# Attention and gated feed-forward on one core: probabilities times values in plain fp32, two heads side by side in PSUM, V loaded one pair ahead, the gate by the sigmoid

## The reference

```python
q_rot, k_rot = rotate(q), rotate(k)                  # rotary embedding
scores = q_rot @ k_rot.T / sqrt(64)
attn = softmax(scores)                               # over the keys
x = attn @ v                                         # 4 x 576 x 512 once the heads are joined
xn = (x - mean) / sqrt(var + 1e-6) * g_ln
x = x + relu(xn @ w_ch1) @ w_ch2                     # 512 -> 2048 -> 512
gate_pre = causal convolution of x over 5 tokens, one weight per tap and feature
out = (1 / (1 + exp(-gate_pre)) * (x @ w_val)) @ w_out
```

## Time and profile before

| | us |
|---|---|
| median of 3 runs | 957.6 (953.64 to 962.07) |
| the profiled execution | 955.4 |
| its span, first to last instruction | 953.5 |

### The profile page before, as it was taken

One profiled execution on the slowest core, in us unless ns is written; L12 is line 12 of the kernel. 1 busy time (PEld: TensorE's weight loads), 2 busy tenths in 40 slices (PEclk: granted clock), 3 DMA queues, 4 the chain that ended last, 5 costly groups with the idle time before them and its releaser, 6 DMA issues.

```text
span 953.5 us, 15415 instructions
## 1 busy us (share of the span) xinstructions
PE 826.4 (87%) x5104; PEld 785.0 (82%) x5104; DVE 579.0 (61%) x967; ACT 385.0 (40%) x927; POOL 251.6 (26%) x193
## 2 busy tenths in 40 slices
PE   0198888989888896399999999999999999999937
PEld 0187777878777785399999999999999999999936
DVE  6587978889798896353276138515732761375074
ACT  1386867778687784222210231122122102311121
POOL 4366768786687820100000000000000000000000
PEclk9999989999899999599999999999999999999977
DMA  8948686766868630541110020011001000100000
GB/s 244 251 119 187 156 180 160 195 164 160 192 148 186 156 87 25 166 148 43 37 32 1 25 76 1 1 56 45 1 13 59 29 1 26 53 1 1 34 0 33
DMA packets 69961, 83.18 MB, mean 87 GB/s; under 512 B 13088, under 2 KB 52256, under 8 KB 69920
## 3 DMA queue, kind: packets, MB, share of 16 engines
q1 hardware_dynamic: 69920, 82.61, 33.7%
HBM read 44.84 MB, written 9.44 MB: 57 GB/s over the span
## 4 chain that ended last, share of the span: by engine, by line
PE 50%; DMA 4%; DVE 3%; issue 1%; POOL 0%; ACT 0%; SPq 0%; DVEq 0%; ACTq 0%
PE ps_y L859 6%; PE ps_y L858 6%; PE ps_y L860 6%; PE ps_h L858 6%; PE ps_h L859 6%; PE ps_h L860 6%; DMA x_tok<-x_scratch 4%; PE ps_ring L858 4%; PE ps_ring L859 3%; PE ps_ring L860 3%; PE ps_ring L870 1%; DVE spare L1014 1%; PE ps_y L880 1%; DVE stats L976 0%; POOL rstd L828 0%
## 5 line engine op out<-in xcount | busy, mean ns | idle before, releaser
L993 DVE SCALAR_TENSOR_TENSOR h_lo<-ps_h,h_hi 128x384 fp32r<-128x384 f32 x96 | 53.2, 554 | 237.8 <-ACT h_hi L936 237.8
L936 ACT ACTIVATE h_hi<-ps_h 128x384 fp32r<-128x384 f32 x96 | 47.2, 492 | 322.8 <-PE ps_h L860 322.8
L410 PE MATMUL ps_scores<-qk 128*128 128x288 f32 (+1 forms) x320 | 104.0, 340 | 71.4 <-DMA qk<-parts 36.9
L585 DVE TENSOR_REDUCE neg_max<-ps_scores 128x1 f32<-128x576 f32 (+1 forms) x160 | 118.7, 750 | 29.3 <-PE ps_scores L411 26.2
L858 PE MATMUL ps_h<-normed_hi,w_hi 128*128 128x384 f32 x384 | 129.8, 338 | 1.4 <-DVE normed_lo L988 1.4
L858 PE MATMUL ps_y<-h_hi,w_hi 128*128 128x384 f32 x384 | 129.8, 338 | 0.0
L860 PE MATMUL ps_h<-normed_hi,w_lo 128*128 128x384 f32 x384 | 129.1, 336 | 0.0
L859 PE MATMUL ps_h<-normed_lo,w_hi 128*128 128x384 f32 x384 | 129.1, 336 | 0.0
L410 PEld LDWEIGHTS ps_scores<-qk 128*128 128x128 f32 (+1 forms) x320 | 59.3, 185 | 84.2 <-ACT probs L505 46.3
L860 PE MATMUL ps_y<-h_hi,w_lo 128*128 128x384 f32 x384 | 128.4, 334 | 0.0
L859 PE MATMUL ps_y<-h_lo,w_hi 128*128 128x384 f32 x384 | 128.3, 334 | 0.0
(11 more groups left out here) (98 smaller groups left out, 1695.6 us busy)
## 6 DMA issues: line engine op xcount, KB each, us to landing
raw<-in_qk SPq DMA_DIRECT2D x16, 576.0 KB, 4.1
swapped<-in_qk SPq DMA_DIRECT2D x64, 144.0 KB, 4.6
qk<-parts SPq DMA_DIRECT2D x32, 256.0 KB, 4.3
x_tok<-x_scratch SPq DMA_DIRECT2D x32, 256.0 KB, 3.2
qk<-parts SPq DMA_DIRECT2D x16, 432.0 KB, 4.0
qk<-parts SPq DMA_DIRECT2D x48, 144.0 KB, 4.2
qk<-parts SPq DMA_DIRECT2D x16, 288.0 KB, 5.2
out_dram<-spare SPq DMA_DIRECT2D x24, 192.0 KB, 1.9
```

The source lines that it names most:

```text
L410: pe.matmul(ps_scores[h][0:rows, c, 0:NC], lhs, qk[par][h][:, 1, cols], start=True, stop=False)
L585: dve.tensor_reduce(neg_max[0:rows, par, t, h:h + 1], ps_scores[h][0:rows, :, 0:NC], AX.XY, ALU.max, negate=True).then_inc(max_ready, 1)
L993: dve.scalar_tensor_tensor(out=h_lo[:, f % 2, :], in0=ps_h[f % 2][:, 0:CH], scalar=0.0, in1=h_hi[:, f % 2, :].bitcast(F32), op0=ALU.max, o ...
```

## The change

- `values` takes both heads at once, for one half of the queries. A product has 64 weight columns (V as it was loaded, fp32) and 288 queries (`pt`, fp32), and writes partitions 0 to 63 of `ps_out` for head 0 and 64 to 127 for head 1. The heads alternate. There are 20 such products a pair in place of 40.
- `part_hi` and `part_lo` become plain copies: HEAD0 by ScalarE (`keep_head0`), HEAD1 and TAILS by VectorE (`keep_head1`). `move_half` and `sum_halves` become one copy on ScalarE (`copy_out`), twice a pair. `values_hi` and `values_lo` are gone, and with them the waits of `prepare` on `v_ready`.
- `load_v` loads the next pair's V rather than that of two pairs ahead; the buffers are two, as before.
- The three orders are written anew: the values of a pair have two steps of 4 products and two of 6.
- The gate is one activation on ScalarE with the function Sigmoid.

```diff
 PE_ORDER = [
-    ("last turn", HEAD1, 3), ("last values", 0, 0), ("last rest", 0, 0),
-    ("scores", 0, 0), ("last turn", TAILS, 3), ("last turn", HEAD0, 4), ("last values", 1, 0),
+    ("last turn", HEAD1, 3), ("last values", 0, 0),
+    ("scores", 0, 0), ("last turn", TAILS, 3), ("last turn", HEAD0, 4), ("last rest", 0, 0),
     ("scores", 1, 0), ("last turn", HEAD1, 4), ("last turn", TAILS, 4),
-    ("scores", 0, 1), ("last rest", 1, 0), ("turn", HEAD0, 0),
+    ("scores", 0, 1), ("turn", HEAD0, 0),
     ("scores", 1, 1), ("turn", HEAD1, 0), ("turn", TAILS, 0),
-    ("scores", 0, 2), ("last values", 0, 1), ("last rest", 0, 1), ("turn", HEAD0, 1),
-    ("scores", 1, 2), ("turn", HEAD1, 1), ("last values", 1, 1),
-    ("scores", 0, 3), ("last rest", 1, 1), ("turn", TAILS, 1),
+    ("scores", 0, 2), ("last values", 1, 0), ("turn", HEAD0, 1),
+    ("scores", 1, 2), ("turn", HEAD1, 1), ("turn", TAILS, 1),
+    ("scores", 0, 3), ("last rest", 1, 0),
     ("scores", 1, 3), ("turn", HEAD0, 2), ("last tokens", 0, 0),
...
 def load_v(pair, par):
-                at_least(sp, v_ready, V_PARTS * (pair - 1))
+                at_least(sp, out_ready, 2 * (pair - 1))
...
-                if not isinstance(pair, int) or pair + 2 < PAIRS:
-                    load_v(pair + 2, par)
+                if not isinstance(pair, int) or pair + 1 < PAIRS:
+                    load_v(pair + 1, 1 - par)
...
             def prepare(j, par):
...
-                at_least(pool, v_ready, V_PARTS * (pair - 1))
...
             prepare(0, 1)
-            values_lo(0, 0)
             with pool.Fori(1, PAIRS // 2) as j:
                 prepare(j, 0)
-                values_lo(2 * j - 1, 1)
                 prepare(j, 1)
-                values_lo(2 * j, 0)
-            values_lo(PAIRS - 1, 1)
...
                 for n in range(2, FULL + 1) if rest else range(2):
-                    lhs = v_both[par][:, 2 * n + h, :] if n < FULL else v_tail[par][h][:, :]
-                    block_ = FULL * h + n if n < FULL else 2 * FULL
-                    pe.matmul(ps_out[:, 0:NC], lhs, pt_hi[:, block_, cols], start=(n == 0), stop=False)
-                    last = pe.matmul(ps_out[:, 0:NC], lhs, pt_lo[:, block_, cols], start=False, stop=(n == FULL))
+                    for h in range(2):
+                        lhs = v_main[par][:, 2 * n + h, :] if n < FULL else v_tail[par][h][:, :]
+                        block_ = FULL * h + n if n < FULL else 2 * FULL
+                        last = pe.matmul(ps_out[h * D:(h + 1) * D, 0:NC], lhs, pt[:, block_, cols],
+                                         start=(n == 0), stop=(n == FULL))
...
+            def copy_out(pair, c):
+                act.wait_ge(out_ready, 2 * pair + c + 1)
+                at_least(act, tokens_turned, 2 * pair)
+                act.copy(o_t[:, c * NC:(c + 1) * NC], ps_out[:, 0:NC]).then_inc(out_copied, 1)
...
-            def exps(c, k):
+            def sigmoid(c, k):
                 act.wait_ge(conv_step, KT * CONV * c + CONV * (k + 1))
-                act.activation(gate[:, k, :], gate[:, k, :], ACT.Exp, scale=-1.0).then_inc(exp_ready, 1)
+                act.activation(gate[:, k, :], gate[:, k, :], ACT.Sigmoid).then_inc(gate_step, 1)
...
-            def sigmoid(c, k):
-                done = 2 * KT * c + 2 * k
-                dve.wait_ge(exp_ready, KT * c + k + 1)
-                dve.tensor_scalar(gate[:, k, :], gate[:, k, :], 1.0, None, ALU.add).then_inc(gate_step, 1)
-                dve.wait_ge(gate_step, done + 1)
-                dve.reciprocal(gate[:, k, :], gate[:, k, :]).then_inc(gate_step, 1)
```

More of the change, by code:

```diff
@@ L53 @@
 ACT_ORDER = [
[L54 to L63, removed]
+    ("exps", 0, 0), ("last turn", HEAD0, 4),
+    ("exps", 1, 0), ("last out", 0, 0),
+    ("exps", 0, 1), ("turn", HEAD0, 0),
+    ("exps", 1, 1),
+    ("exps", 0, 2), ("turn", HEAD0, 1),
+    ("exps", 1, 2), ("last out", 1, 0),
+    ("exps", 0, 3),
+    ("exps", 1, 3), ("turn", HEAD0, 2),
+    ("exps", 0, 4),
+    ("exps", 1, 4), ("turn", HEAD0, 3),
 ]
@@ L66 @@
     ("scores", 0, 0), ("last turn", HEAD1, 3), ("last turn", TAILS, 3),
[L67 to L76, removed]
+    ("scores", 1, 0), ("last turn", HEAD1, 4),
+    ("scores", 0, 1), ("last turn", TAILS, 4),
+    ("scores", 1, 1), ("turn", HEAD1, 0),
+    ("scores", 0, 2), ("turn", TAILS, 0),
+    ("scores", 1, 2), ("turn", HEAD1, 1),
+    ("scores", 0, 3), ("turn", TAILS, 1),
+    ("scores", 1, 3), ("last tokens", 0, 0), ("turn", HEAD1, 2),
+    ("scores", 0, 4), ("turn", TAILS, 2), ("last tokens", 1, 0),
+    ("scores", 1, 4),
 ]
@@ L200, in attention @@
         inv = sb("inv", [P, NQ, 2])
-        half = sb("half", [P, NC])
         o_t = sb("o_t", [P, S])
@@ L238, in attention @@
         PREP = 6
-        V_PARTS = 3
+        V_LOADS = 3 * 16
         LOADS = 5 * 16
@@ L465, in walk @@
                         turn(pair, par, x, y)
-                    elif kind == "values":
-                        values(pair, par, x, y)
                     elif kind == "last turn":
@@ L470, in walk @@
                     elif kind == "last values":
-                        values(before, pb, x, y)
-                    elif kind == "rest":
-                        values(pair, par, x, y, rest=True)
+                        values(before, jb, pb, x)
                     elif kind == "last rest":
-                        values(before, pb, x, y, rest=True)
+                        values(before, jb, pb, x, rest=True)
                     elif kind == "last tokens":
@@ L488, in _ @@
             act.wait_ge(cleared_sums, 1)
-            def values_hi(pair, j, par):
-                act.wait_ge(v_loaded[par], 48 * (j + 1))
-                at_least(act, out_ready, 4 * (pair - 1))
-                apart(act, passed)
-                act.copy(v_both[par][:, :, 0:D], v_raw[par][:, :, :]).then_inc(v_hi_ready, 1)
-                for h in range(2):
-                    rows = slice(h * D, (h + 1) * D)
-                    act.copy(v_tail[par][h][rows, 0:D], v_raw_tail[par][rows, :]).then_inc(v_hi_ready, 1)
             def exps(pair, par, h, t):
@@ L503, in exps @@
                 act.wait_ge(max_ready, UNITS * pair + 2 * t + h + 1)
+                if h == 0:
+                    at_least(act, turned, GROUPS * pair + 3 * (t - 1))
+                    apart(act, passed)
                 p = probs[(par * NQ + t) % 2]
@@ L966, in _ @@
             run(act, {"slab": slab_part, "evict": evict, "up": relu, "keep": keep, "split": part_x,
-                      "sigmoid": exps, "gated parts": part_gated, "project": copy_out})
+                      "sigmoid": sigmoid, "gated parts": part_gated, "project": copy_out})
         @block.vector
@@ L1040, in _ @@
             run(dve, {"slab": slab_part, "stats": take_stats, "scale": scale, "evict": evict, "up": relu,
-                      "split": part_x, "conv": conv, "sigmoid": sigmoid, "gated": gated, "gated parts": part_gated})
+                      "split": part_x, "conv": conv, "gated": gated, "gated parts": part_gated})
 def program(nc, qk, v, cos, sin, ident, g_ln, w_ch1, w_ch2, w_val, conv_w, w_out, out):
```

118 lines of the change are left out of this document (43 added, 75 removed).

## The result

| | before | after |
|---|---|---|
| median of the runs, us | 958.08 (953.64 to 962.07, 4 runs) | 911.44 (907.43 to 914.28, 4 runs) |
| ratio, 95% interval | | 0.951 (0.945 to 0.957) |
| profiled execution, us | 955.4 | 914.28 |
| its span, us | 953.5 | 912.5 |
| first scores of pair 1 / pair 15 | 60.25 / 348.44 | 60.01 / 325.99 |

What follows compares the result with a forecast made beforehand. Attention was taken as bound by a two-pair loop through V, 20.0 us a pair. 955.4 - 32.5 (pairs 1 to 15) - 4.7 (rest of attention) - 10 (gate) = 908, so 910 for the median; range 893 to 986.

Steps and rivals of the forecast that it cites:

- The loop through V: Attention before: V split, V on POOL, prepare, stack and landing form a two-pair loop, 40.1 us, 20.0 a pair.
- The walk of 18.1: Time of one attention pair after the change, summed as 13.4 - 1.2 + 5.1 + 0.8 us.
- of the 1.2 us in which PE idles I take all away: Attention walk: lighter VectorE and ScalarE work removes all 1.2 us of TensorE idle time in a pair.
- The products: 5.1 plus 0.8: The 20 new values products take 5.1 us a pair, eight changes between 128 and 64 columns 0.8 more.
- The four streams: Values step: one plain fp32 product of 288 columns costs four streams through the array, 0.49 to 0.53 us.
- The overlap: Values step: both heads' products run in the array at once, 4.9 to 5.3 us a pair instead of 9.8 to 10.6.
- No overlap: Rival, chance 0.32: the two heads' values products follow each other; walk 22.6 us, total 982.
- In part: Rival, chance 0.14: only one head's last pass meets the other's first; walk 20.5 us, total 948.
- The supply binds: Rival, chance 0.10: supply of q and k, at least 17.0 us a pair, binds instead of V; walk 19.5, total 930.
- V one pair ahead, and the copies: Attention: loading V one pair ahead costs nothing; VectorE's copies cost the same as the subtractions they replace.
- Clock and feed-forward: Half-clock spells in attention cost 6 us before, 3 left; the feed-forward before its last keep was forecast unchanged.
- The gate: -10: End of the feed-forward: one Sigmoid on ScalarE beside the next convolution starts the last gated 10 us earlier.

Runs made afterwards that it cites:

- before_no_add: Kernel before with VectorE's addition of 1e-9 to the softmax sums left out: 962.85 us, 1.005 of before.
- v_split_early: Kernel before with ScalarE's split of V moved up, to behind the copies of tile 0: 954.15 us, 0.997 of before.
- no_add: Changed kernel with VectorE's addition of 1e-9 to the softmax sums left out: 898.53 us, 0.940 of before.
- one_column: no_add with all products but the last key tile's in the same half of the array: 958.74 us, 1.002 of before.
- wide: no_add with each product taking V of both heads as 128 weight columns: 961.33 us, 1.004 of before.
- floor: no_add with only 8 of the 20 products of a walk made: 889.51 us, 0.930 of before.
- v_once: no_add with V loaded for two pairs only and used again by the later pairs: 897.85 us.
- before_sigmoid: Kernel before with only the gate changed to one Sigmoid activation: 946.27 us, 0.990 of before.
- v_split_no_add: v_split_early with the addition of 1e-9 to the softmax sums also left out: 929.67 us, 0.972 of before.
- by_head: Changed kernel with the products of a step ordered by head instead of alternating: 934.9 us, 0.979 of before.

## Why the prediction was right, step by step

**The loop through V bounds the kernel before, at 20.0.** Right, but not alone. before_no_add keeps the 40.0 in the two neighbouring walks at full clock, and v_split_early, which cuts the loop, loses the alternation of 21 and 19. What I had not seen is the second bound at 20.4, tokens behind VectorE's addition, which made the cut alone worth 3 us. The change cut the loop and shortened VectorE's and TensorE's work in one, so the second bound came out lower too, at 19.0.

**The walk of 18.1.** The forecast was 13.4 - 1.2 + 5.1 + 0.8. no_add measures 18.0, with 0.3 of idle time left: this is the walk if TensorE hardly waits. In the kernel after it was 19.0. The step that failed is the one that said "of the 1.2 us in which PE idles I take all away": 1.1 us a walk stayed. Of these 15.0 us in fourteen walks (265.98 - 251.01), 10.5 are the wait behind the addition, which was to be seen in the trace of before: 1179 ns for ten columns, beside 217 for the reciprocal of the same size. I had looked only for the costliest groups.

**The products: 5.1 plus 0.8.** Measured 5.4 in all. The four streams are right: 0.49 for a product without a partner (one_column, wide). The overlap is right: 0.24 with one. The changes of width are smaller, 0.15 for a pair, 0.6 a walk. The Trainium skill (FP8 and Floating Point Precision, TensorE Precision Notes) gives true fp32 four passes through the array. The 0.49 agrees, as four times 0.12, though the trace records two instructions of 0.24 and not four.

**The rivals.** "No overlap" was put at 982, with a walk of 22.6. Its mechanism was run as one_column, on the kernel without the addition: 958.7 with a walk of 21.8. There one product in each half of the queries still overlaps, 2 x 0.49 a walk; without that a walk would be 22.8 and the time, an estimate from these two, 958.7 + 16 x 0.98 = 974, before the addition is put back. So the rival's price was sound; what failed in it is the condition, since the heads do overlap. "In part" got its reason wrong: TensorE does not stop at the first instruction whose columns are busy. "The supply binds" has its 17 us (floor), one microsecond below the walk of no_add; in the kernel after it did not bind.

**V one pair ahead, and the copies.** V costs nothing (v_once). The copies of VectorE take 681 ns where the subtractions took 682. Over the fourteen walks VectorE is busy for 13.1 us a walk, within the 12.5 to 14.5 of the forecast, and ScalarE for 11.0, 4.9 less than before where I had said 5.5. The group of the kernel after:

```profile
L556 DVE COPY pt<-ps_turn 128x512 f32<-128x512 f32 x64 | 43.6, 681 | 1.0 <-PE ps_turn L402 1.0
```

**Clock and feed-forward.** I left 3 us for spells at the lower level and there were none, which gave back a quarter of what the addition took. The feed-forward before its last `keep` became 3.0 shorter where I had forecast nothing: half of it comes with the gate (before_sigmoid), so the additions and reciprocals beside a full PE were probably not quite free, though no run shows where they held it up; the other half stays open.

**The gate: -10.** Measured -11.1 as a change of its own, -11.4 in the last stage.

**What the products as such bring.** v_split_no_add (18.6 a walk) and no_add (18.0) differ by the products, the copies and the place of V's loads. That is 8 us in fourteen walks, when neither the loop nor the addition binds. With the addition in place the shares are others: cutting the loop alone (v_split_early) takes 3.3 of the 22.2 us that fourteen walks lose, and the other 19 come only with the lighter work of TensorE and VectorE. So one can't say what part of the 41 us is the products'; only the gate's, 11 to 13, stands by itself. The saving that one would read out of the diff (40 products for 20) is small in any case: 5.6 us a walk were forecast to become 5.9 and became 5.4.

## What to carry to other kernels

When two bounds lie within half a microsecond (here 20.0 and 20.4 a walk), an edit that lifts one of them measures as almost nothing; lift both before dropping either. A short VectorE instruction whose time varies tenfold (look at least, median and most, not at the sum) is waiting for something that no semaphore shows. Products of two 64-column halves need not alternate strictly, but here the partner had to be within four instructions; and work that fills the waits between scores should stay in small steps.

## What the runs showed of the hardware

- A matmul with plain fp32 operands, 288 columns, is two instructions of 0.24 us each at 2.4 GHz, whether it has 64 (one_column) or 128 weight columns (wide); two of 64 columns in different halves run at the same time, 0.27 a product with the changes of width (after).
- TensorE starts matmuls out of program order: the seventh instruction with the third, when the ones between use the other columns (by_head, 203.14; the step of twelve takes 2.14). The Trainium skill (TensorE: Matmul & The Clock Gate, Part 2, Step-by-step) lets only weight loads go ahead and has the matmuls themselves stay in program order. The measurement differs from the page here, and it decides.
- VectorE's `tensor_scalar` on 128x10 fp32 in SBUF takes 0.16 us or up to 2.44, until GpSimd's running instruction ends (after); `reciprocal` on the same ten columns takes 0.205 to 0.207 always (no_add). The Trainium skill (SBUF — State Buffer, Who interferes with whom) says that VectorE in a two-port mode, which `tensor_scalar` can enter, and GpSimd lock a port pair for a whole instruction. The trace agrees in its times, 285.05 against 285.02; that the addition runs in such a mode no view shows.
